# Windowed attention ahead of two feed-forward blocks: dilated heads in 32 x 64 blocks, and three attention steps in one place of the instruction order

## The reference

```python
B, H, S, D = 4, 8, 576, 64
scores = (1 / sqrt(D)) * q @ k.T
rel = pos[:, None] - pos[None, :]
mask_plain = (rel >= 0) & (rel < 32)                       # heads 0 to 3
mask_dil = (rel >= 0) & (rel < 128) & (rel % 4 == 0)       # heads 4 to 7
attn = softmax(where(mask, scores, -1e9));  x = attn @ v   # rows of all heads side by side: (4, 576, 512)

xk = mu_k * x + (1 - mu_k) * x_prev;  xr = mu_r * x + (1 - mu_r) * x_prev
x = sigmoid(xr @ w_r) * (relu(xk @ w_k) ** 2 @ w_v)        # 512 -> 1024 -> 512

u = x + (relu(x.T @ w_tok1) @ w_tok2).T                    # over tokens: 576 -> 256 -> 576
out = u + relu(u @ w_ch1) @ w_ch2                          # over channels: 512 -> 1536 -> 512
```

## Time and profile before

| | us |
|---|---|
| median of three runs | 697.4 (697.18 to 698.02) |
| the profiled execution | 699.19 |
| its span, first to last instruction | 697.4 |
| TensorE busy | 688.9 (99%) |
| VectorE / ScalarE / GpSimd busy | 365.0 / 236.6 / 202.1 |
| mean granted TensorE clock | 0.997 of full speed |

### The profile page before, as it was taken

One profiled execution on the slowest core, in us unless ns is written; L12 is line 12 of the kernel. 1 busy time (PEld: TensorE's weight loads), 2 busy tenths in 40 slices (PEclk: granted clock), 3 DMA queues, 4 the chain that ended last, 5 costly groups with the idle time before them and its releaser, 6 DMA issues.

```text
span 697.4 us, 14338 instructions
## 1 busy us (share of the span) xinstructions
PE 688.9 (99%) x5777; PEld 615.3 (88%) x5777; DVE 365.0 (52%) x623; ACT 236.6 (34%) x546; POOL 202.1 (29%) x238
## 2 busy tenths in 40 slices
PE   8999999999999999999999999999999999999997
PEld 7879999999999999999888888888788888888886
DVE  5689867686867677686763136221462125311121
ACT  4574653626454453545521122111231122111110
POOL 6274645747464655643073000000000000000000
PEclk9999999999999999999999999999999999999999
DMA  9861332332332330342721311403112221300011
GB/s 202 214 187 42 53 69 51 61 58 55 73 63 57 55 72 23 80 70 84 279 49 22 56 25 55 67 14 64 60 32 39 41 35 61 63 6 1 0 61 31
DMA packets 179729, 45.85 MB, mean 66 GB/s; under 512 B 167880, under 2 KB 172112, under 8 KB 179664
## 3 DMA queue, kind: packets, MB, share of 16 engines
q1 hardware_dynamic: 175424, 43.71, 28.2%
q10 hardware_dynamic: 4240, 1.23, 1.0%
HBM read 30.22 MB, written 4.72 MB: 50 GB/s over the span
## 4 chain that ended last, share of the span: by engine, by line
PE 98%; ACT 1%; DVE 0%; issue 0%; POOL 0%; DVEq 0%; POOLq 0%; ACTq 0%
PE bank L956 13%; PE bank L958 12%; PE bank L957 12%; PE tq L956 8%; PE tq L958 8%; PE tq L957 8%; PE s L1528 4%; PE s L1527 4%; PE s L1526 4%; PE bank L1527 3%; PE bank L1528 3%; PE bank L1526 3%; PE bank L1011 2%; PE bank L823 2%; PE s L602 1%; PE bank L1071 1%
## 5 line engine op out<-in xcount | busy, mean ns | idle before, releaser
L1518 DVE SCALAR_TENSOR_TENSOR h_lo<-bank,h_hi 128x512 fp32r<-128x512 f32 (+1 forms) x30 | 19.0, 638 | 100.7 <-ACT h_hi L1512 100.6
L1518 DVE SCALAR_TENSOR_TENSOR h_lo<-tq,h_hi 128x512 fp32r<-128x512 f32 (+1 forms) x30 | 18.9, 637 | 99.0 <-ACT h_hi L1512 99.0
L1051 POOL TENSOR_TENSOR k_lo<-kr,k_hi 128x288 fp32r<-128x288 f32 x64 | 55.1, 864 | 25.8 <-ACT k_hi L1047 25.7
L1093 DVE RECIPROCAL rg<-rg 128x288 f32<-128x288 f32 x32 | 61.4, 1923 | 0.0
L1512 ACT ACTIVATE h_hi<-tq 128x512 fp32r<-128x512 f32 (+1 forms) x30 | 16.7, 557 | 118.7 <-PE bank L1528 97.0
L1512 ACT ACTIVATE h_hi<-bank 128x512 fp32r<-128x512 f32 (+1 forms) x30 | 16.7, 557 | 118.0 <-PE bank L1528 93.4
L956 PE MATMUL bank<-k_hi,WV_hi 128*128 128x288 f32 x184 | 56.0, 304 | 0.0
L957 PE MATMUL bank<-k_hi,WV_lo 128*128 128x288 f32 x184 | 54.2, 295 | 0.0
L958 PE MATMUL bank<-k_lo,WV_hi 128*128 128x288 f32 x184 | 54.1, 294 | 0.0
L1528 PE MATMUL s<-C_hi,h_lo 128*128 128x512 f32 x120 | 47.5, 396 | 0.0
L1526 PE MATMUL s<-C_hi,h_hi 128*128 128x512 f32 x120 | 47.1, 393 | 0.3 <-DVE urows L1555 0.3
(11 more groups left out here) (242 smaller groups left out, 1993.9 us busy)
## 6 DMA issues: line engine op xcount, KB each, us to landing
C_raw<-in_moe_w_ch SPq DMA_DIRECT2D x6, 1024.0 KB, 11.2
urows<-blocks SPq DMA_DIRECT2D x64, 64.0 KB, 2.1
out_x<-urows SPq DMA_DIRECT2D x16, 256.0 KB, 2.0
vt<-in_v SPq DMA_DIRECT2D x70, 48.0 KB
qraw<-in_q SPq DMA_DIRECT2D x128, 24.0 KB, 2.0
kraw<-in_k SPq DMA_DIRECT2D x128, 24.0 KB, 1.9
xraw<-blocks SPq DMA_DIRECT2D x48, 64.0 KB, 2.1
vt<-in_v SPq DMA_DIRECT2D x7, 320.0 KB, 3.7
```

The costliest lines, as they stand in the source:

```text
L1051: e.tensor_tensor(lo, t, hi.bitcast(F32), ALU.subtract).then_inc(Z.lo_done, 1)
L1093: e.reciprocal(t, t).then_inc(Z.r_done, 1)
L1518: e.scalar_tensor_tensor(lo, ps[:, 0:w], 0.0, hi.bitcast(F32), ALU.max, ALU.subtract).then_inc(Z.h2l_done, 1)
```

## The change

The dilated doubles get the plain block form. The 48 queries of a residue are split into 32 and 16 (QU), each with 64 keys; the second block begins 16 keys (B0) later. Per dilated double the scores become 32 matmuls of 32 queries and 64 keys instead of 16 of 64 and 80, the turn four transposes of 128x128 instead of eight of 112x80, its copy one activation instead of four, the values 32 matmuls (32 or 16 columns, 64 keys deep) instead of 16 of 48 columns, 80 keys deep. Softmax tiles have 512 instead of 640 elements a partition. v of a dilated double comes in four DMAs instead of one, since each of the two blocks and each head parity has its own rows in SBUF. The 1e-9 of the sum is added by an instruction of its own, as for plain doubles. The masks take ten instructions on GpSimd instead of six.

From double 10 on a double starts every 35/6 units. The turn of n stands where the scores of n + 1 stand, and the values of n where the scores of n + 2 stand, so that in one unit come scores of n, values of n - 2 and turn of n - 1. The last doubles are treated apart. Double 23 begins in unit 106 instead of 118.

```diff
-QB, KB = 48, 48 + WINDOW
+QB = 48
-GC = 4 * KB
-KS = KB + 1
 QP, KP = 32, 32 + WINDOW
+QU = ((0, QP), (QP, QB))
+B0 = QB - QP
-GS = 4 * KS
+GS = 4 * KP
...
         def v_loads(n):
             if n % 2:
-                return 2 if n == 3 else 1
+                return 4
             return 8 if where(n)[1] else 12
...
+        def load_dilated(e, n, u, h, landed):
+            b, j, _ = where(n)
+            k0 = QB * j - WINDOW + B0 * u
+            skip = B0 if u else WINDOW if j == 0 else 0
+            rows = key_rows(u, h)
+            vs = v[b, H // 2:H, :, :].rearrange("(s h) (i r) d -> h i s (r d)", h=2, r=DIL)[h]
+            e.dma_start(dilated_v(n, slice(rows.start + skip, rows.stop), u), vs[k0 + skip:k0 + KP]).then_inc(landed, 16)
...
-                k0 = QB * j - WINDOW
-                skip = WINDOW if j == 0 else 0
-                groups_ = [(0, 2), (2, 2)] if n == 3 else [(0, 4)]
-                for h0, nh in groups_:
-                    vs = v[b, 4 * dil + h0:4 * dil + h0 + nh, :, :]
...
-                    e.dma_start(dst(slice(skip, KB)),
-                                vs.rearrange("h (i r) d -> i h (r d)", r=DIL)[k0 + skip:k0 + KB]).then_inc(landed, 16)
+                for u in range(2):
+                    for h in range(2):
+                        load_dilated(e, n, u, h, landed)
...
-                for s in range(2):
-                    for g in range(2):
-                        for a in range(2):
-                            c = 2 * g + a
-                            q0 = 256 * s + 64 * c if n < NPE else SU * s + QB * c
-                            for h in range(2):
-                                rows = slice(64 * h, 64 * h + 64)
-                                c0 = 512 * h + KB * (2 * s + g)
-                                last = e.matmul(s2[64 * a:64 * a + 64, c0:c0 + KB],
-                                                qT[rows, q0:q0 + 64], keys(rows, s, c),
-                                                start=True, stop=True)
+                for m in range(16 if dil else 2 * NP):
+                    g, a = divmod(m, 4)
+                    s, c = divmod(m // 2, DIL) if dil else divmod(m, NP)
+                    u = m % 2
+                    for h in range(2):
+                        rows = slice(64 * h, 64 * h + 64)
+                        c0 = 512 * (h ^ u) + KP * g
+                        last = e.matmul(s2[QP * a:QP * (a + 1), c0:c0 + KP], queries(rows, s, c, u), keys(rows, s, c, u),
+                                        start=True, stop=True)
...
-                for g in range(4):
-                    last = e.transpose(ps[0:KB, TR * g:TR * (g + 1)], sb[0:TR, GS * h + KS * g:GS * h + KS * g + KB],
-                                       ident[0:TR, 0:TR])
-                last.then_inc(Z.pb_done if h else Z.pa_done, 1)
+                for g in range(ngroups(n) // 2):
+                    last = e.transpose(ps[:, P * g:P * (g + 1)], sb[:, P * g:P * (g + 1)], ident[:, :])
+                last.then_inc(Z.pa_done, 1)
...
-                e.activation(dst[:, 0], src[:, :, 0:QB], ACT.Copy)
-                e.activation(dst[:, 1], src[:, :, 64:TR], ACT.Copy).then_inc(Z.ptb_done if h else Z.pta_done, 1)
+                e.activation(p_buffer(n)[:, 0:w], p_bank(n)[:, 0:w], ACT.Copy).then_inc(Z.pta_done, 1)
...
+                for m in range(16 if n % 2 else 2 * NP):
+                    s, c = divmod(m // 2, DIL) if n % 2 else divmod(m, NP)
+                    u = m % 2
+                    i0, i1 = QU[u] if n % 2 else (0, QP)
...
-        STARTS = [5 * (n - 4) if n <= 9 else 25 + 20 * (n - 9) // 3 for n in range(4, ND)]
+        STARTS = [5 * (n - 4) if n <= 9 else 25 + 35 * (n - 9) // 6 for n in range(4, ND)]
...
-                late[t + 7].append(p_transpose(n, 0))
-                early[t + 8].append(p_evict(n, 0))
-                late[t + (8 if n < NPE else 7)].append(p_transpose(n, 1))
-                early[t + (9 if n < NPE else 8)].append(p_evict(n, 1))
-                tv = STARTS[n - 3] + 2 if NPE < n < ND - 1 else t + 9
+                if NPE + 1 < n < ND - 1:
+                    tp, tv = STARTS[n - 3] + 2, STARTS[n - 2] + 2 if n < ND - 2 else STARTS[n - 3] + 7
+                    values[tp].append(p_transpose(n))
+                else:
+                    tp, tv = t + 7, STARTS[n - 3] + 2 if NPE < n < ND - 1 else t + 9
+                    late[tp].append(p_transpose(n))
+                early[tp + 1].append(p_evict(n))
```

More of the change, by code:

```diff
@@ L647, in vector @@
                 if dil:
[L648 to L651 removed]
+                    m = masks[:, 0:KP] if j else masks[:, KP:2 * KP]
+                    m = m.unsqueeze(1).unsqueeze(1).broadcast_to([P, 2, 4, KP])
+                    dst = sb[:, 0:8 * KP].rearrange("p (g h x) -> p h g x", g=4, h=2)
+                    src = banks[:, :, 0:4 * KP].rearrange("p h (g x) -> p h g x", g=4)
                 else:
@@ L816, in tensor @@
-                for s in range(2):
-                    o_ = o_bank(n, s)
-                    if (n, s) == (3, 1):
-                        e.wait_ge(Z.x_done, 2)
-                    for c in range(DIL):
-                        for h in range(2):
-                            p0 = 2 * SU * h + SU * s + QB * c
-                            last = e.matmul(o_[64 * h:64 * h + 64, SU * s + QB * c:SU * s + QB * (c + 1)],
-                                            raw_v(n, slice(0, KB), 2 * s + h)[:, D * c:D * (c + 1)],
-                                            p_buffer(n)[0:KB, p0:p0 + QB], start=True, stop=True)
+                if n == 3:
+                    e.wait_ge(Z.mu_done, 1)
@@ new lines, in tensor @@
+                wait(e, Z.x_done, n - 1 if n in (1, 2, 3) else n)
+                if n in (0, 7, 8):
+                    e.wait_ge(Z.q_done, 8 if n else 4)
+                elif n in (4, 5, 6):
+                    e.wait_ge(Z.k_done, n + 2)
+                for m in range(16 if n % 2 else 2 * NP):
+                    s, c = divmod(m // 2, DIL) if n % 2 else divmod(m, NP)
+                    u = m % 2
+                    i0, i1 = QU[u] if n % 2 else (0, QP)
+                    o0 = SU * s + QB * c + i0 if n % 2 else QP * m
+                    for h in range(2):
+                        rows = key_rows(u, h)
+                        value = dilated_v(n, rows, u)[:, s, D * c:D * (c + 1)] if n % 2 else plain_v(n, rows, s)[:, u, c // 2]
+                        last = e.matmul(o_bank(n, u)[64 * h:64 * h + 64, o0:o0 + i1 - i0], value,
+                                        p_buffer(n)[rows, QP * m:QP * m + i1 - i0], start=True, stop=True)
@@ L838, in x_evict, with o_part @@
+        def o_part(n, u):
+            rows = o_bank(n, u)[:, 0:2 * SU]
+            if n % 2:
+                return rows.rearrange("p (s r i) -> p s r i", s=2, r=DIL)[:, :, :, QU[u][0]:QU[u][1]]
+            return rows.rearrange("p (s e u q) -> p u s e q", s=2, u=2, q=QP)[:, u]
         def x_evict(n):
[L839 removed]
             def scalar(e):
                 e.wait_ge(Z.o_done, n + 1)
[L843 to L854 removed]
+                for u in range(1 if n in (2, 3) else 2):
+                    last = e.activation(x_part(n, u), o_part(n, u), ACT.Copy)
```

251 lines of the change are left out of this document (76 added, 175 removed).

## The result

Median of four runs 723.6 us (723.0 to 726.7), the kernel before beside it 697.7; ratio 1.038, 95% interval 1.034 to 1.041. The forecast was 717.7, range 707 to 726. The profiled execution is the slowest of the four, 726.7, span 724.9.

The account below looks back on a forecast made before the run. TensorE bounds the kernel, and SyncE's issue queue, nearly without slack, would set the changed one: scores of double 23 at 271.9, plus 425.3 after them, 19.2 for 12 units and 1.3 of attention, give 717.7 us; range 707 to 726.

Parts of the forecast that it names:

- What bounds: TensorE busy 688.9 of 697.4 us; SyncE's queue issues without a gap, its loads only 3.4 us faster per six doubles.
- Part 1: What TensorE executes in the dilated doubles: shorter groups of small matmuls and transposes, -2.5 us in all.
- Part 2: The prologue: longer scores, shorter turns, more DMA issues; no sign that dominates, 0, from -1 to +1 us.
- Part 3, a dilated v: SyncE's queue: four issues of 0.55 us instead of one of 0.49, 1.7 us more per dilated double.
- Part 3, q and k: SyncE's queue: last q and k issued at about 267 us, scores of double 23 at 271.9.
- one long issue: SyncE's queue ahead of double 23: +1.0 us added for a longer stretch and more instruction fetches.
- The way after double 23: From the scores of 23 to the end: 425.3 us, plus 19.2 for 12 units and 1.3 more of attention.
- Rival A: Faster: SyncE's queue does not bind, only TensorE's shorter groups count, 694.9 us; chance 0.07.
- the change of tiling mode: TensorE: the skill says it drains the engine, so fewer, longer groups gain more; a turn costing only 0.1 us extra opposed it.
- Rival B: More than the queue: VectorE's catching up and TensorE's clock falling in waits add +2 to +8, about 723 us; chance 0.16.
- The waits themselves: TensorE waiting in scores, idle about 20 us between 100 and 272 us.
- The waits of VectorE: At block_transposes, for DMA of q or k, largest at even doubles, 15 to 25 us in all.

Follow-up runs that it names:

- b_v4: The kernel before with v of each dilated double from 9 on in four DMAs of a quarter of its rows instead of one; 698.5 us.
- b_new: The kernel before with only the starts changed, 35/6 units apart instead of 20/3 from the tenth double on; 707.3 us.
- a_form: The changed kernel with starts, turn and values placed as before; new blocks and dilated v in four DMAs stay; 712.4 us.
- a_act: The changed kernel with the k loads of doubles 10 to 23 issued from ScalarE's queue instead of SyncE's; 700.8 us.
- a_actform: a_form with the k loads of doubles 10 to 23 issued by ScalarE; 699.8 us.
- a_wk: a_actform with the first two loads of w_k issued behind v of doubles 0 and 1, and behind v of 2; 701.3 us.
- a_warm: a_actform with the prologue's filling matmuls a third as many and three times as long; 699.7 us.
- b_wk: The kernel before with the first two loads of w_k issued behind v of doubles 0 and 1, and behind v of 2; 700.2 us.

## Why the prediction was right, and where it was off

The mechanism, the sign and the range held. The single number did not: 723.6 is 5.9 us above 717.7 and outside the forecast's own 712 to 721.

- **What bounds (right).** The queue of SyncE had 3.4 us to spare per six doubles. b_v4 used them up without a loss, b_new and a_form went over, and a_act took the loss away. Between the same place of two batches (v of a dilated double, 157.21 and 239.12 us) the changed kernel's queue takes 81.9 us, for 79.5 forecast.
- **Part 1 (right).** Forecast -2.5 us; measured -2.2 in a_act (661.4 against 663.6). A place takes nearly what I said. Even doubles, between the last large matmul ahead and the second behind:

```profile
128.41 0.29 PE L885 MATMUL tq<-xk_lo,WK_hi 128*128 128x288 f32 x1
128.63 0.73 PE L607 MATMUL s<-kT,qT 64*32 64x64 f32 x48
...
130.12 0.66 PE L719 MATMUL bank<-ident,sm 128*128 128x128 f32 x4
130.53 0.38 PE L883 MATMUL bank<-xk_hi,WK_hi 128*128 128x288 f32 x1
130.75 0.29 PE L884 MATMUL bank<-xk_hi,WK_lo 128*128 128x288 f32 x1
```

2.34 us less the two steps of 0.13 is 2.08, for a forecast of 1.95; odd ones came to 2.32 for 2.35. Where the gain comes from is another matter: I wrote that "the smaller blocks hardly matter", but a_actform, which has the blocks and not the places, already has all of it (660.9 against 663.6), and places and starts add nothing. The four transposes instead of eight are the gain: a turn takes 0.44 us instead of 0.79 to 0.91, while scores and values of a pair take 3.73 instead of 3.51.
- **Part 2 (wrong).** "I find no sign that dominates: 0": it was +3.7 us in this profile and +2.4 to +6.7 in the others with the new blocks. I had counted the DMAs and let them go, and had not asked what TensorE's own instructions cost; the 0.72 us of "issue" in the old prologue was the row to ask about. It is half of what the forecast missed in this profile (3.7 of 7.2 us), with the reservation above on single profiles.
- **Part 3, a dilated v (right).** Four issues with gaps take 2.4 us, in some doubles 1.9, less 0.49: +1.4 to +1.9 for a forecast of 1.7.
- **Part 3, q and k (mis-sized).** The q and k of sixteen doubles take 143.1 us of issue against 138.7, +4.4; I had put one long issue, 1.0, and that is the term that was mis-sized. The last issue begins at 275.7, not at about 267, which had no long issue in it: 3.5 of the difference come from the start (69.20 against 65.68), 4.4 from here, the rest from v. Why long issues are more frequent is not shown.
- **The way after double 23 (right).** 445.5 us for 445.8.
- **Rival A (not seen).** SyncE's rows show no gap. What I set against the change of tiling mode proves nothing, though: the turn in the earlier trace rows has the tiles of the large matmuls, 128*128.
- **Rival B (its number, not its mechanism).** It had about 723, and 723.6 came: that is luck. The clock did fall behind the waits (7.4 us of slower work), but in time that TensorE would have waited anyway, as the prediction says of most of it, and the way from 23 on was as long as forecast. What brought the time up was the prologue and the issues of q and k. The waits themselves (18.5 us) were near the 20 that I gave.
- **Sum.** 717.7 became 724.9 in the profile: prologue +3.7, to the scores of 23 +3.7, rest -0.3. The waits of VectorE (35.1 us) are nearly twice what I gave; it has slack of its own, and only 16.8 us reach TensorE.

## What to carry to other kernels

Before moving users of loads earlier, compare how long the issuing queue and the users need for one period: when the queue's rows follow one another without a gap, the time of issue is the supply, and a spare of 3 us in 78 is gone with a few more DMAs. Relieving such a queue (an issue on another engine) costs nothing in bytes and is to be tried ahead of any finer placement. Splitting small matmuls finer can be cheap (here 64 more instructions in the scores and values of a pair cost 0.2 us), but each is an instruction to fetch, and in a prologue that fills the DMA engines this shows.

## What the runs showed of the hardware

- The issue of a DMA depends on its shape: 0.34 to 0.41 us with 12 or 20 rows of four heads (b_v4), 0.60 with 64 rows of two heads, 0.43 or 0.59 with 48, 0.43 with 32, and 0.44 with 32 rows for q and k.
- TensorE stopped without a semaphore after its 219th matmul in nearly every kernel (0.3 to 3.9 us), for instructions that came through the same, full DMA engines as the data; less traffic ahead of them shortened the stop to 0.28 us (a_wk), fewer instructions to 0.46 (a_warm).
- Behind each of the twelve longest waits of TensorE in these profiles (2.7 to 5.1 us) the granted clock was 0.50 for 2 us or more; of the shorter ones some were followed by it (1.4 us in the changed kernel) and others not (2.1 us in b_wk). Whether that costs time depends on what follows: 7.4 us of slower work in the changed kernel went into waits that would have been there anyway.
